# Listed tokens of a fused attention and mixture-of-experts kernel: column groups over strided blocks, 32x32 turns on VectorE

## The chip, the cores and the metric

One core of a Trainium2 chip runs the whole program. The metric is the device time of one execution in microseconds (us); lower is better.

## The reference

Three stages follow each other; the output of each is the input of the next.

```
# 1. attention with a memory term: B=2, H=8, S=576, D=64
a = softmax(causal(q @ k.T / sqrt(D)));  local = a @ v
mem_out = (phi(q) @ M_prev) / (phi(q) . z_prev)
x = g * mem_out + (1 - g) * local            # -> 1152 tokens x 512
# 2. dense layer: w_in 512x2048, w_out 2048x512
h = x @ w_in
g = where(h >= 1, h, where(h <= -1, 0, (h + 1)**2 / 4))
x2 = g @ w_out                               # 1152 x 512
# 3. experts, one per token: w1 8x512x1024, w2 8x1024x512, capacity 288 tokens each
e = argmax(x2 @ w_gate);  gate = max(softmax(x2 @ w_gate))
out[i] = gate * (relu(x2[i] @ w1[e]) @ w2[e])   # tokens over an expert's capacity give 0
```

## The kernel before

Activations are held with features on the 128 partitions and tokens along the free side. Stage 1 goes over 8 pairs of heads, stage 2 over four chunks of 288 tokens, each of eight steps of two 128-feature tiles. The products of the first chunk, and of the expert that runs first, are made of three FP32R products each (high and low parts); the others are plain FP32.

With these inputs nearly all tokens choose one expert, that of token 0. Its first 288 tokens are the first chunk, and they go through that expert as a block: `main_first` (w1) and `main_second` (w2), eight tiles `f` each, in lines 2076 to 2097. The tokens that chose another expert are few. Their numbers come out of a small product (`list_tokens`, line 2127) as a list of up to 32, and these are the "listed tokens". They are computed again from their attention result in rows of 32:

- `all_slots` apart, the queue of GpSimd (POOL) fetches the 32 rows of 512 numbers from `x_d` in device memory (line 844). `x_d` was written earlier by `store_rows` (line 605), by 32x32-turned pieces.
- `few_x` (line 2143) turns the 32x512 rows to four 128x32 tiles with TensorE; ScalarE (ACT) copies them to `x_fewT`.
- `few_hidden` (line 2151) multiplies by `w_in`. The 32 tokens are the stationary operand, 128x32, and the weights stream past. The array is used in four column groups of 32: group `g` writes partitions 32g to 32g+31 of a bank. Group `g` takes the columns 512g to 512g+511 of the 2048, so that all four groups run side by side.
- VectorE (DVE) and ACT apply the piecewise function to the 128x512 result (lines 1634, 1091, 1092, 1636).
- `few_turned` (line 2161) turns it with four TensorE transposes, and ACT copies the result to `g_fewT` (line 1094).
- The product with `w_out` (line 2187) has a quarter of the 2048 contraction rows in each group, 512 columns wide, so that four partial sums lie on the four groups of 32 partitions. DVE copies them (line 1640), and TensorE sums the four and turns them with `sel`, four identities of 32 stacked (line 2196). DVE copies that to `x2_fewT`.
- For three experts `k` (the first one and two others): `few_first` (w1, group g takes the columns 256g to 256g+255 of 1024), ACT's ReLU with the gate (zero for tokens of another expert), `few_turn` (two TensorE transposes), ACT's copy to `h_fewT`, `few_second` (w2, group g takes the columns 128g to 128g+127), all three experts summed in one bank.
- DVE copies the bank to `y_few` and POOL scatters it to the output in pieces of 128 columns (line 875).

The order of all this is written out by hand in each engine's instruction stream. On TensorE `few_x` stands after `main_second(4)`, `few_hidden` after `main_second(5)`, `few_turned` in the middle of `main_second(7)`, and the rest at the end, with the turns of the block's result (`expert_rows`, line 2099) for the first 288 tokens put in between. On the sync engine (SP) the weights of the second other expert are requested once `few_hidden` has ended (line 629).

A part for more than two other experts or more than 32 listed tokens (`work`) is skipped at run time by a count in a register; with these inputs it does not run.

Of the kernel before, what the change touches and what calls it, by code (L numbers as in the profile page):

```python
# [4 lines left out]
F32 = mybir.dt.float32  # L5
F32R = mybir.dt.float32r
BF16 = mybir.dt.bfloat16
I32 = mybir.dt.int32
# [5 lines left out]
def build_program(nc, q, k, v, m_prev, z_prev, beta, w_in, w_out, w_gate, w1, w2, out, capacity):  # L14
# [13 lines left out]
    N = B * S  # L28
# [26 lines left out]
    with ctx:  # L55
# [155 lines left out]
        few_row, _, _ = sb("few_row", [FEW, 1], I32)  # L211
# [33 lines left out]
        x_few, _, _ = sb("x_few", [FEW, DM], F32)  # L245
# [5 lines left out]
        g_fewT, _, _ = sb("g_fewT", [P, FG, P], F32)  # L251
# [3 lines left out]
        x2_few, _, _ = sb("x2_few", [P, DM], F32)  # L255
        x2_fewT, _, _ = sb("x2_fewT", [P, DT, FEW], F32)
        h_few = [sb(f"h_few{k}", [P, F_PART], F32)[0] for k in range(OTHERS + 1)]
        h_fewT = [sb(f"h_fewT{k}", [P, 2, P], F32)[0] for k in range(OTHERS + 1)]
# [130 lines left out]
        s_fpos = sem("s_fpos")  # L389
        s_fx = sem("s_fx")  # L390
        s_ft = sem("s_ft")
# [6 lines left out]
        s_fgt = sem("s_fgt")  # L398
# [5 lines left out]
        s_kt2 = sem("s_kt2")  # L404
# [124 lines left out]
        def _(sp):  # L529
# [75 lines left out]
            def store_rows(j):  # L605

                sp.wait_ge(s_xre, j + 1)
                b, m = divmod(j, KT)
                for a in range(4):
                    sp.dma_start(x_d[b * S:(b + 1) * S, m * P + 32 * a:m * P + 32 * a + 32].rearrange("(g t) c -> t g c", t=32),  # L610
                                 x_rows[j % 2][32 * a:32 * a + 32, :].rearrange("t (g c) -> t g c", c=32)).then_inc(s_xst[j % 2], 16)
# [60 lines left out]
        k_banks = ((bank_pt[0], bank_pt[1], bank_t), (f_bank[0], f_bank[1], f_bank[2]))  # L672
# [11 lines left out]
        def _(pool):  # L684
# [156 lines left out]
            for n in range(2):  # L841
                pool.wait_ge(s_xst[n], 16 * 4 * NPAIR // 2)
            pool.wait_ge(s_fid, 1)
            pool.indirect_dma_start(out=x_few[:, :], out_offset=None, in_=x_d[:, :],
                                    in_offset=bass.IndirectOffsetOnAxis(ap=few_row[:, 0:1], axis=0),
                                    bounds_check=N - 1, oob_is_err=False).then_inc(s_fx, 16)
# [35 lines left out]
        def _(act):  # L882
# [205 lines left out]
            act.wait_ge(s_ft, 1)  # L1088
            act.activation(x_fewT[:, :, :], bank_t[:, 128:256].rearrange("p (m w) -> p m w", w=FEW), ACT.Copy).then_inc(s_fte, 1)
# [3 lines left out]
            act.wait_ge(s_fgt, 1)  # L1093
            act.activation(g_fewT[:, :, :], bank_pt[1][:, :].rearrange("p (b w) -> p b w", w=P), ACT.Copy).then_inc(s_fgte, 1)
# [3 lines left out]
            def few_relu(k):  # L1098

                act.wait_ge(s_kh, k + 1)  # L1100
                act.wait_ge(s_fid, 6)
                act.activation(h_few[k][:, :], k_banks[0][k][:, 0:F_PART], ACT.Relu, scale=few_gate[:, k:k + 1]).then_inc(s_khe, 1)

            def few_turned(k):

                act.wait_ge(s_kt2, k + 1)
                act.activation(h_fewT[k][:, :, :], k_banks[1][k][:, 0:F_PART].rearrange("p (b w) -> p b w", w=P),
                               ACT.Copy).then_inc(s_kte, 1)
# [3 lines left out]
            for k in range(OTHERS + 1):  # L1112
                few_turned(k)
# [15 lines left out]
        def _(dve):  # L1129
# [173 lines left out]
            def clear_counts():  # L1303
# [6 lines left out]
                dve.tensor_copy(parts[:, :, 4:5].rearrange("p r a -> p (r a)"), tok_f[:, 0:1].to_broadcast([ST, NTOK])).then_inc(s_seen, 1)  # L1310
                dve.tensor_reduce(sel[:, :], ident[:, :].rearrange("p (g w) -> p w g", w=32), AX.X, ALU.add
# [283 lines left out]
            def rows_out(J, gates):  # L1595

                for r in range(slot_tiles):
                    dve.wait_ge(s_er, slot_tiles * J + r + 1)
                    dve.tensor_scalar(y_row[r][:, :], row_banks[r][0:ST, :], gates(r), None, ALU.mult).then_inc(s_ere, 1)

            dve.wait_ge(s_list, 1)
# [15 lines left out]
            for g in range(GROUPS):  # L1617
                dve.tensor_scalar(few_t[FEW * g:FEW * (g + 1), :], tab_tok[FEW * g:FEW * (g + 1), :], float(GROUPS), float(g - NOWHERE),
                                  ALU.mult, ALU.add).then_inc(s_fpos, 1)
# [8 lines left out]
            dve.wait_ge(s_fpos, GROUPS)  # L1628
# [45 lines left out]
        def _(pe):  # L1674
# [468 lines left out]
            def few_x():  # L2143

                pe.wait_ge(s_fx, 16)
                for m in range(KT):
                    last = pe.transpose(bank_t[:, 128 + m * FEW:128 + (m + 1) * FEW], x_few[:, m * P:(m + 1) * P],
                                        ident[0:FEW, 0:FEW])
                last.then_inc(s_ft, 1)

            def few_hidden():
# [9 lines left out]
            def few_turned():  # L2161

                pe.wait_ge(s_fg, 1)
                for b in range(FG):
                    last = pe.transpose(bank_pt[1][:, b * P:(b + 1) * P], g_few[:, b * P:(b + 1) * P], ident[:, :])
                last.then_inc(s_fgt, 1)
# [6 lines left out]
            for f in range(ET - 1):  # L2173
# [12 lines left out]
            assert FT == 4 * GROUPS  # L2186
# [102 lines left out]
```

## Time and profile before

| | us |
|---|---|
| median of 3 runs (310.83 to 311.3) | 310.91 |
| the profiled execution | 310.3 |
| its span, first to last instruction in the trace | 308.4 |
| TensorE (PE) busy | 301.0 (98%) |
| PE weight load (PEld) busy | 247.6 (80%) |
| VectorE (DVE) busy | 216.1 (70%) |
| ScalarE (ACT) busy | 153.0 (50%) |
| GpSimd (POOL) busy | 136.5 (44%) |

The profiled execution took 310.3 us, of which 1.9 us lie outside the span. The mean TensorE clock granted was 0.997 of full speed. L2190 in a row is line 2190 of the kernel before. A plain FP32 product appears as two MATMUL records, so that the 16 products of line 2190 are x32.

### The profile page before, as it was taken

Reading aid. Unit: us, or ns where it says so; the run is one execution under the profiler, and the core shown is the slowest. Engines: PE = TensorE matmul, PEld = TensorE weight load, DVE = VectorE, ACT = ScalarE, POOL = GpSimd, SP = SyncE. Lnnn points to the kernel's source line nnn. Section 1 sums busy time; section 2 is a strip of 40 time slices with the busy share of each in tenths; the row PEclk is TensorE's granted clock in tenths of the full one; section 3 lists DMA queues with packets and bytes.
Section 4 is the critical chain, followed back from the end, with each engine's and each line's share of the span. In section 5 each row is a group of like instructions: output and inputs, shape, how many; then the busy total and the mean of one; then the engine's idle time right before and its main releaser. Section 6 shows DMA issues by size and latency. Waiting matters only on the chain.

```text
span 308.4 us, 7108 instructions
## 1 busy us (share of the span) xinstructions
PE 301.0 (98%) x2747; PEld 247.6 (80%) x2747; DVE 216.1 (70%) x574; ACT 153.0 (50%) x337; POOL 136.5 (44%) x154
## 2 busy tenths in 40 slices
PE   7999999999999999999999999999999999999993
PEld 6666676666677988887999989898989899995573
DVE  2999998999977366997884567956775588852300
ACT  1796875867866144655551353446354556301130
POOL 4878997998997300564781012014021333110121
PEclk9999999999999999999999999999999999999998
DMA  7989897861447600000000409660025039079940
GB/s 162 156 192 235 205 207 157 199 187 31 154 119 183 197 2 0 2 2 0 2 0 8 71 3 351 213 98 3 0 38 79 2 99 429 19 255 378 402 145 9
DMA packets 75047, 38.48 MB, mean 125 GB/s; under 512 B 66008, under 2 KB 66016, under 8 KB 73988
## 3 DMA queue, kind: packets, MB, share of 16 engines
q1 hardware_dynamic: 72340, 36.74, 44.9%
q10 hardware_dynamic: 2416, 0.59, 0.9%
q0 software_dynamic: 256, 0.67, 0.7%
q8 instruction: 23, 0.38, 0.5%
q14 instruction: 12, 0.10, 0.1%
HBM read 32.66 MB, written 5.39 MB: 123 GB/s over the span
## 4 chain that ended last, share of the span: by engine, by line
PE 94%; POOL 2%; DVE 1%; issue 1%; ACT 0%; POOLq 0%
PE bank_a L1846 17%; PE bank_b L1846 17%; PE bank_out L1803 6%; PE bank_a L1702 4%; PE bank_b L1906 4%; PE bank_pt L1906 4%; PE bank_pt L1754 4%; PE bank_a L1780 3%; PE bank_out L1800 2%; PE bank_a L2085 2%; PE bank_out L1879 2%; PE bank_b L2085 2%; PE bank_b L1697 2%; PE bank_out L2225 2%; PE bank_b L2095 2%; PE bank_a L2095 2%
## 5 line engine op out<-in xcount | busy, mean ns | idle before, releaser
L722 POOL TENSOR_SCALAR prob<-prob,rl,gate_loc 128x512 f32<-128x512 f32 (+3 forms) x64 | 41.5, 663 | 11.0 <-DVE rl L1243 11.0
L1846 PE MATMUL bank_a<-x_hi,win_hi 128*128 128x288 f32 x128 | 39.3, 307 | 0.0
L1846 PE MATMUL bank_b<-x_hi,win_hi 128*128 128x288 f32 x128 | 38.2, 298 | 0.0
L1846 PE MATMUL bank_b<-x_lo,win_hi 128*128 128x288 f32 x128 | 38.1, 297 | 0.0
L1846 PE MATMUL bank_b<-x_hi,win_lo 128*128 128x288 f32 x128 | 38.0, 297 | 0.0
L1846 PE MATMUL bank_a<-x_hi,win_lo 128*128 128x288 f32 x128 | 38.0, 297 | 0.0
L1846 PE MATMUL bank_a<-x_lo,win_hi 128*128 128x288 f32 x128 | 38.0, 297 | 0.0
L973 ACT ACTIVATE g_raw<-bank_a,biases 128x576 f32<-128x576 f32 x16 | 11.9, 742 | 49.5 <-DVE sq L1320 49.5
L910 ACT ACTIVATE prob<-prob,negmax 128x512 f32<-128x512 f32 (+3 forms) x64 | 35.0, 550 | 0.3 <-DVE negmax L1193 0.3
L806 POOL TENSOR_TENSOR w_lo<-w_sb,w_hi 128x512 fp32r<-128x512 f32 x8 | 11.3, 1414 | 48.3 <-ACT w_hi L1016 48.3
L751 POOL TENSOR_TENSOR x_lo<-xT,x_hi 128x1152 fp32r<-128x1152 f32 x4 | 10.6, 2661 | 48.7 <-ACT x_hi L923 48.7
L1326 DVE TENSOR_TENSOR g_raw<-g_raw,sq 128x576 f32<-128x576 f32 x32 | 31.5, 985 | 0.5 <-ACT sq L974 0.5
L1846 PEld LDWEIGHTS bank_a<-x_hi,win_hi 128*128 128x128 f32 x128 | 24.2, 189 | 3.5 <-issue 3.4
L1320 DVE TENSOR_SCALAR sq<-bank_a 128x576 f32<-128x576 f32 x16 | 12.0, 752 | 21.2 <-PE bank_a L1846 21.2
L819 POOL TENSOR_TENSOR wo_lo<-wout,wo_hi 128x512 fp32r<-128x512 f32 x16 | 22.1, 1392 | 10.5 <-ACT wo_hi L989 10.5
L1846 PEld LDWEIGHTS bank_b<-x_hi,win_hi 128*128 128x128 f32 x128 | 24.2, 189 | 0.5 <-issue 0.5
L974 ACT ACTIVATE sq<-sq,biases 128x576 f32<-128x576 f32 x32 | 24.5, 766 | 0.0
L1846 PEld LDWEIGHTS bank_a<-x_lo,win_hi 128*128 128x128 f32 x128 | 24.1, 189 | 0.0
L1846 PEld LDWEIGHTS bank_b<-x_lo,win_hi 128*128 128x128 f32 x128 | 24.1, 188 | 0.0
L1846 PEld LDWEIGHTS bank_a<-x_hi,win_lo 128*128 128x128 f32 x128 | 24.1, 188 | 0.0
L1846 PEld LDWEIGHTS bank_b<-x_hi,win_lo 128*128 128x128 f32 x128 | 24.1, 188 | 0.0
L973 ACT ACTIVATE g_raw<-bank_b,biases 128x576 f32<-128x576 f32 x16 | 11.9, 741 | 20.1 <-DVE sq L1320 20.1
(333 smaller groups left out, 796.7 us busy)
## 6 DMA issues: line engine op xcount, KB each, us to landing
w_sb<-in_moe_w_dram SPq DMA_DIRECT2D x6, 2048.0 KB, 11.2
win_raw<-in_moe_w_in_dram SPq DMA_DIRECT2D x4, 1024.0 KB, 5.7
wout<-in_moe_w_out_dram SPq DMA_DIRECT2D x4, 1024.0 KB, 5.5
win_raw<-in_moe_w_in_dram SPq DMA_DIRECT2D x1, 4096.0 KB, 13.3
out_dram<-zero_row SPq DMA_DIRECT2D x8, 288.0 KB
x_d<-x_rows SPq DMA_DIRECT2D x32, 72.0 KB, 2.1
v_sb<-in_v_dram SPq DMA_DIRECT2D x16, 128.0 KB, 2.5
qn<-in_q_dram SPq DMA_DIRECT2D x24, 72.0 KB, 5.4
```

The source lines that it names most:

```text
L722: pool.tensor_scalar(prob[u][:, h, :], prob[u][:, h, :], rl[:, c:c + 1], gate_loc[:, 2 * j + h:2 * j + h + 1], ALU.mult, ALU.mult).then_in ...
L819: pool.tensor_tensor(wo_lo[:, f % WSLOTS, :], wout[:, f, :], wo_hi[:, f % WSLOTS, :], ALU.subtract).then_inc(s_wol, 1)
L910: last = act.activation(p, p, ACT.Exp, scale=-1.0, bias=negmax[:, c:c + 1], accum_out=rsum[:, c:c + 1])
L973: act.activation(g_raw[:, 2 * d:2 * d + 2, :], h_bank(d), ACT.Relu, bias=biases[:, 1:2]).then_inc(s_re, 1)
L974: act.activation(sq[d % 2][:, :, :], sq[d % 2][:, :, :], ACT.Square, scale=0.5, bias=biases[:, 0:1]).then_inc(s_sq, 1)
L1326: dve.tensor_tensor(g_raw[:, two, :], g_raw[:, two, :], sq[d % 2][:, :, :], ALU.add).then_inc(s_g, 1)
L1702: last = pe.matmul(s_part(u, h), qT[i % 2][part, u * P:(u + 1) * P], kT[i % 2][part, 0:(u + 1) * P], start=True, stop=True)
L1754: last = pe.transpose(dst[:, c * P:(c + 1) * P], prob[u][:, h, c * P:(c + 1) * P], ident[:, :])
L1803: last = pe.matmul(bank_t[part, c * P:NFULL * P], v_sb[j % 2][:, c, h, :], probT[:, h, c * KSTEP + c * P:c * KSTEP + NFULL * P], start=Fal ...
L1846: last = pe.matmul(h_bank(d)[:, t, :], w[:, m, f:f + P], x[c % 2][:, m, :], start=(m == 0 and n == 0), stop=(m == KT - 1 and n == 2))
L1906: last = pe.matmul(y_bank[m], w[:, f % WSLOTS, part], x, start=(f == 0 and n == 0), stop=(f == FT - 1 and n == 2))
L2085: last = pe.matmul(e_bank(f)[:, 0:SLOTS], w, x[:, m, :], start=(m == 0 and n == 0), stop=(m == DT - 1 and n == 2))
```

## The change

What it does, for the listed tokens alone:

- A column group `g` no longer takes a contiguous quarter of the columns, but every fourth run of 32 columns: the runs g, g+4, g+8 and so on. `strided()` gives this view of the moving operand, and the bank is written contiguously as before. If a 128-partition result of this form is turned in 32x32 blocks, it stands directly with the contraction features on the partitions.
- So the three TensorE turns (`few_x`, `few_turned`, `few_turn`) and the sum with `sel` go. In their place come 32x32-block transposes by VectorE: `x_fewT` (128x128), `g_fewT` (128x512), `x2_fewT` (128x128, from PSUM) and three of `h_fewT` (128x256). The ACT copies go too.
- The product with `w_out` has all 16 tiles of the contraction in every group and 128 columns in each, in place of 4 tiles and 512 columns: 64 products of 128 columns in place of 16 of 512.
- The fetch of the rows reads 128 pieces of 128 numbers in place of 32 rows of 512, with index 4 * token + group (`of_group`, made by eight small memsets while the first chunk runs). `few_t` is one instruction in place of four. For the block order to come out, `store_rows` writes its 32-column pieces to other columns of `x_d`.
- On TensorE the three tiles of `expert_rows` stand together behind the product with `w_out`.
- `work` turns its rows by four times as many products (not run here).

```diff
@@ SP, store_rows
-                    sp.dma_start(x_d[b * S:(b + 1) * S, m * P + 32 * a:m * P + 32 * a + 32].rearrange("(g t) c -> t g c", t=32),
+                    sp.dma_start(x_d[b * S:(b + 1) * S, a * P + 32 * m:a * P + 32 * m + 32].rearrange("(g t) c -> t g c", t=32),
@@ POOL
-            pool.indirect_dma_start(out=x_few[:, :], out_offset=None, in_=x_d[:, :],
+            quarters = x_d.rearrange("n (a w) -> (n a) w", a=GROUPS)
+            pool.indirect_dma_start(out=x_few[:, :], out_offset=None, in_=quarters[:, :],
                                     in_offset=bass.IndirectOffsetOnAxis(ap=few_row[:, 0:1], axis=0),
-                                    bounds_check=N - 1, oob_is_err=False).then_inc(s_fx, 16)
+                                    bounds_check=GROUPS * N - 1, oob_is_err=False).then_inc(s_fx, 16)
@@ ACT
-            act.wait_ge(s_ft, 1)
-            act.activation(x_fewT[:, :, :], bank_t[:, 128:256].rearrange("p (m w) -> p m w", w=FEW), ACT.Copy).then_inc(s_fte, 1)
...
-            act.wait_ge(s_fgt, 1)
-            act.activation(g_fewT[:, :, :], bank_pt[1][:, :].rearrange("p (b w) -> p b w", w=P), ACT.Copy).then_inc(s_fgte, 1)
...
-            for k in range(OTHERS + 1):
-                few_turned(k)
@@ DVE, first chunk
+                for g in range(GROUPS):
+                    for n, value in enumerate((float(g), float(g - NOWHERE))):
+                        dve.memset(of_group[FEW * g:FEW * (g + 1), n:n + 1], value).then_inc(s_group, 1)
@@ DVE, listed tokens
-            dve.scalar_tensor_tensor(out=few_row[:, :], in0=tab_few[0:FEW, 3:4], scalar=float(ST), in1=tab_few[0:FEW, 4:5],
-                                     op0=ALU.mult, op1=ALU.add).then_inc(s_fid, 1)
             dve.scalar_tensor_tensor(out=tab_tok[:, :], in0=tab_few[:, 3:4], scalar=float(ST), in1=tab_few[:, 4:5],
                                      op0=ALU.mult, op1=ALU.add).then_inc(s_tab, 1)
+            dve.wait_ge(s_tab, 2)
+            dve.scalar_tensor_tensor(out=few_row[:, :], in0=tab_tok[:, :], scalar=float(GROUPS), in1=of_group[:, 0:1],
+                                     op0=ALU.mult, op1=ALU.add).then_inc(s_fid, 1)
...
+            dve.wait_ge(s_fx, 16)
+            dve.transpose(x_fewT[:, :, :].rearrange("p m w -> p (m w)"), x_few[:, :]).then_inc(s_fte, 1)
             dve.wait_ge(s_fh, 1)
             dve.tensor_scalar(c_few[:, :], bank_pt[0][:, :], -1.0, 1.0, ALU.max, ALU.min).then_inc(s_fc, 1)
             dve.wait_ge(s_fsq, 1)
             dve.tensor_tensor(g_few[:, :], g_few[:, :], c_few[:, :], ALU.add).then_inc(s_fg, 1)
+            dve.wait_ge(s_fg, 1)
+            dve.transpose(g_fewT[:, :, :].rearrange("p t w -> p (t w)"), g_few[:, :]).then_inc(s_fgte, 1)
             copy_yt(0, 0)
             copy_yt(0, 1)
             dve.wait_ge(s_f2, 1)
-            dve.tensor_copy(x2_few[:, :], bank_o[:, :]).then_inc(s_f2e, 1)
+            dve.transpose(x2_fewT[:, :, :].rearrange("p m w -> p (m w)"), bank_o[:, 0:P]).then_inc(s_f2e, 1)
-            row_out(0)
-            dve.wait_ge(s_f2, 2)
-            dve.tensor_copy(x2_fewT[:, :, :], f_bank[3][:, 0:P].rearrange("p (m w) -> p m w", w=FEW)).then_inc(s_f2e, 1)
-            for r in range(1, slot_tiles):
+            for r in range(slot_tiles):
                 row_out(r)
+            for k in range(OTHERS + 1):
+                dve.wait_ge(s_khe, k + 1)
+                dve.transpose(h_fewT[k][:, :, :].rearrange("p f w -> p (f w)"), h_few[k][:, :]).then_inc(s_kte, 1)
@@ PE
+            def strided(w, g):
+                return w.rearrange("p (t g c) -> p g t c", g=GROUPS, c=FEW)[:, g, :, :]
 
             def few_hidden():
...
-                        last = pe.matmul(bank_pt[0][FEW * g:FEW * (g + 1), :], x_fewT[:, m, :], win_raw[:, m, DM * g:DM * (g + 1)],
-                                         start=(m == 0), stop=(m == KT - 1))
+                        last = pe.matmul(bank_pt[0][FEW * g:FEW * (g + 1), :].rearrange("p (t c) -> p t c", c=FEW), x_fewT[:, m, :],
+                                         strided(win_raw[:, m, :], g), start=(m == 0), stop=(m == KT - 1))
...
-                if f == 4:
-                    few_x()
...
-            main_second(ET - 1, range(2))
-            few_turned()
-            main_second(ET - 1, range(2, DT))
+            main_second(ET - 1, range(DT))
             pe.wait_ge(s_fgte, 1)
-            for i in range(FT // GROUPS):
+            for f in range(FT):
                 for g in range(GROUPS):
-                    f = GROUPS * i + g
-                    last = pe.matmul(bank_o[FEW * g:FEW * (g + 1), :], g_fewT[:, f % FG, FEW * (f // FG):FEW * (f // FG + 1)],
-                                     wout[:, f, :], start=(i == 0), stop=(i == FT // GROUPS - 1))
+                    last = pe.matmul(bank_o[FEW * g:FEW * (g + 1), 0:P].rearrange("p (t c) -> p t c", c=FEW), g_fewT[:, f, :],
+                                     strided(wout[:, f, :], g), start=(f == 0), stop=(f == FT - 1))
             last.then_inc(s_f2, 1)
-            expert_rows(0, range(2))
+            expert_rows(0, range(slot_tiles))
             pe.wait_ge(s_f2e, 1)
-            for m in range(DT):
-                last = pe.matmul(f_bank[3][:, FEW * m:FEW * (m + 1)], x2_few[:, m * P:(m + 1) * P], sel[:, :], start=True, stop=True)
-            last.then_inc(s_f2, 1)
-            pe.wait_ge(s_fid, 2)
-            expert_rows(0, range(2, slot_tiles))
-            pe.wait_ge(s_f2e, 2)
...
-                        last = pe.matmul(k_banks[0][k][FEW * g:FEW * (g + 1), 0:F_PART], x2_fewT[:, m, :],
-                                         w1_sb[k][:, m, F_PART * g:F_PART * (g + 1)], start=(m == 0), stop=(m == DT - 1))
+                        last = pe.matmul(k_banks[k][FEW * g:FEW * (g + 1), 0:F_PART].rearrange("p (t c) -> p t c", c=FEW),
+                                         x2_fewT[:, m, :], strided(w1_sb[k][:, m, :], g), start=(m == 0), stop=(m == DT - 1))
...
-            for k in range(OTHERS + 1):
-                few_turn(k)
```

## Rows read from the trace of the kernel before

**Rows 1.** The page's chain that ended last, share of the span by engine.

```profile
PE 94%; POOL 2%; DVE 1%; issue 1%; ACT 0%; POOLq 0%
```

**Rows 2.** The chain in order of time from 262 us on: start us, us, what.

```profile
275.81 0.36 PE bank_out L2147 x4
276.17 0.99 PE bank_a L2095 x6
277.17 0.80 PE bank_b L2095 x6
277.97 3.62 PE bank_pt L2157 x32
...
281.61 0.70 DVE c_few L1634
...
282.33 0.69 ACT g_few L1091
...
283.66 0.70 DVE g_few L1636
...
284.41 0.66 PE bank_pt L2165 x4
285.07 0.80 PE bank_b L2095 x6
285.86 3.57 PE bank_out L2190 x32
289.43 1.01 PE bank_a L2104 x8
290.44 0.89 PE bank_b L2196 x8
291.33 0.45 PE bank_b L2104 x4
291.78 3.59 PE bank_pt L2207 x64
295.37 1.73 PE bank_out L2207 x32
297.10 0.59 PE bank_a L2216 x4
...
297.69 0.44 PE bank_b L2216 x2
298.13 5.59 PE bank_out L2225 x192
...
303.75 0.30 DVE y_few L1653
```

**Rows 3.** TensorE's timeline: start us, us, engine line, tiles.

```profile
285.79 3.64 PE L2190 MATMUL bank_out<-wout,g_fewT 128*32 128x512 f32 x32
```

**Rows 4.** VectorE's groups by form: busy us, mean ns, idle before.

```profile
L1337 DVE STREAM_TRANSPOSE w_turn<-wout 128x1024 f32<-128x1024 f32 x8 | 9.8, 1229 | 0.0
...
L1348 DVE STREAM_TRANSPOSE wp<-bank_out 128x512 f32<-128x512 f32 x1 | 0.7, 703 | 0.0
```

**Rows 5.** SP's timeline from 255 us on: start of the last weight requests.

```profile
281.74 0.37 SPq L599 DMA_DIRECT2D w_sb<-in_moe_w_dram  x1
282.21 0.46 SPq L603 DMA_DIRECT2D w_sb<-in_moe_w_dram  x1
```

**Rows 6.** Tile w_sb from 255 us on: the four requests' time to landing.

```profile
DMA to landing us min/median/max: 8.6/11.4/14.2
```

**Rows 7.** DMA issues, 220 to 309 us: median us to landing.

```profile
x_few<-x_d,few_row POOLq DMA_INDIRECT x1, 3.3
```

**Rows 8.** POOL's timeline: the fetch of the listed rows.

```profile
269.01 1.60 POOL L844 DMA_INDIRECT x_few<-x_d,few_row  x1 [11.70 <-DVE few_row L1604]
```

**Rows 9.** VectorE's timeline in the first chunk.

```profile
112.14 0.06 DVE L1306 MEMSET seen<- 96x4 uint32 x1
...
115.49 0.76 DVE L1320 TENSOR_SCALAR sq<-bank_a 128x576 f32<-128x576 f32 x1 [0.49 <-PE bank_a L1846]
```

More of the change, by code:

```diff
@@ L210, in build_program @@
         few_id, _, _ = sb("few_id", [P, 1], I32)
-        few_row, _, _ = sb("few_row", [FEW, 1], I32)
+        few_row, _, _ = sb("few_row", [P, 1], I32)
+        of_group, _, _ = sb("of_group", [P, 2], F32)
         job_id, _, _ = sb("job_id", [ST, NR], I32)
@@ L244, in build_program @@
         hT, _, _ = sb("hT", [P, ET, SLOTS], F32, at=phase)
-        x_few, _, _ = sb("x_few", [FEW, DM], F32)
+        x_few, _, _ = sb("x_few", [P, DM_PART], F32)
         x_fewT, _, _ = sb("x_fewT", [P, KT, FEW], F32)
@@ L250, in build_program @@
         c_few, _, _ = sb("c_few", [P, DM], F32)
-        g_fewT, _, _ = sb("g_fewT", [P, FG, P], F32)
+        g_fewT, _, _ = sb("g_fewT", [P, FT, FEW], F32)
         assert offset[0] <= reused
@@ L254, in build_program @@
         y_row = [sb(f"y_row{r}", [ST, DM], F32)[0] for r in range(slot_tiles)]
-        x2_few, _, _ = sb("x2_few", [P, DM], F32)
         x2_fewT, _, _ = sb("x2_fewT", [P, DT, FEW], F32)
         h_few = [sb(f"h_few{k}", [P, F_PART], F32)[0] for k in range(OTHERS + 1)]
-        h_fewT = [sb(f"h_fewT{k}", [P, 2, P], F32)[0] for k in range(OTHERS + 1)]
+        h_fewT = [sb(f"h_fewT{k}", [P, ET, FEW], F32)[0] for k in range(OTHERS + 1)]
         assert offset[0] <= later_at
@@ L389, in build_program @@
         s_fpos = sem("s_fpos")
+        s_group = sem("s_group")
         s_fx = sem("s_fx")
-        s_ft = sem("s_ft")
         s_fte = sem("s_fte")
@@ L397, in build_program @@
         s_fg = sem("s_fg")
-        s_fgt = sem("s_fgt")
         s_fgte = sem("s_fgte")
@@ L403, in build_program @@
         s_khe = sem("s_khe")
-        s_kt2 = sem("s_kt2")
         s_kte = sem("s_kte")
@@ L670, in s_part @@
             return s_bank(u)[:, 512 * h + at:512 * h + at + (u + 1) * P]
-        k_banks = ((bank_pt[0], bank_pt[1], bank_t), (f_bank[0], f_bank[1], f_bank[2]))
+        k_banks = (bank_pt[0], bank_pt[1], bank_t)
         NGROUP = DM // P
@@ L1101, in few_relu @@
                 act.wait_ge(s_fid, 6)
[L1102 to L1108, printed above, removed]
+                act.activation(h_few[k][:, :], k_banks[k][:, 0:F_PART], ACT.Relu, scale=few_gate[:, k:k + 1]).then_inc(s_khe, 1)
             for k in range(OTHERS + 1):
                 few_relu(k)
-            for k in range(OTHERS + 1):
-                few_turned(k)
             def work(n):
@@ L1599, in rows_out @@
                     dve.tensor_scalar(y_row[r][:, :], row_banks[r][0:ST, :], gates(r), None, ALU.mult).then_inc(s_ere, 1)
+            dve.wait_ge(s_group, 2 * GROUPS)
             dve.wait_ge(s_list, 1)
@@ L1616, in _ @@
             dve.wait_ge(s_tab, 3)
-            for g in range(GROUPS):
-                dve.tensor_scalar(few_t[FEW * g:FEW * (g + 1), :], tab_tok[FEW * g:FEW * (g + 1), :], float(GROUPS), float(g - NOWHERE),
-                                  ALU.mult, ALU.add).then_inc(s_fpos, 1)
+            dve.scalar_tensor_tensor(out=few_t[:, :], in0=tab_tok[:, :], scalar=float(GROUPS), in1=of_group[:, 1:2],
+                                     op0=ALU.mult, op1=ALU.add).then_inc(s_fpos, 1)
             second_lo(6)
@@ L1627, in _ @@
             dve.wait_ge(s_fid, 4)
-            dve.wait_ge(s_fpos, GROUPS)
+            dve.wait_ge(s_fpos, 1)
             dve.tensor_tensor(few_at[:, :], few_any[:, :], few_t[:, :], ALU.mult).then_inc(s_fid, 1)
@@ L2141, in name_jobs @@
                 pe.matmul(sum_ps, biases[0:E, 1:2], col[:, 4:6], start=True, stop=True).then_inc(s_name, 1)
[L2143 to L2149, printed above, removed]
+            def strided(w, g):
+                return w.rearrange("p (t g c) -> p g t c", g=GROUPS, c=FEW)[:, g, :, :]
             def few_hidden():
@@ L2156, in few_hidden @@
                     for g in range(GROUPS):
-                        last = pe.matmul(bank_pt[0][FEW * g:FEW * (g + 1), :], x_fewT[:, m, :], win_raw[:, m, DM * g:DM * (g + 1)],
-                                         start=(m == 0), stop=(m == KT - 1))
+                        last = pe.matmul(bank_pt[0][FEW * g:FEW * (g + 1), :].rearrange("p (t c) -> p t c", c=FEW), x_fewT[:, m, :],
+                                         strided(win_raw[:, m, :], g), start=(m == 0), stop=(m == KT - 1))
                 last.then_inc(s_fh, 1)
[L2161 to L2166, printed above, removed]
             pe.wait_ge(s_xh, 1)
@@ L2206, in few_first @@
                     for g in range(GROUPS):
-                        last = pe.matmul(k_banks[0][k][FEW * g:FEW * (g + 1), 0:F_PART], x2_fewT[:, m, :],
-                                         w1_sb[k][:, m, F_PART * g:F_PART * (g + 1)], start=(m == 0), stop=(m == DT - 1))
+                        last = pe.matmul(k_banks[k][FEW * g:FEW * (g + 1), 0:F_PART].rearrange("p (t c) -> p t c", c=FEW),
+                                         x2_fewT[:, m, :], strided(w1_sb[k][:, m, :], g), start=(m == 0), stop=(m == DT - 1))
                 last.then_inc(s_kh, 1)
-            def few_turn(k):
-                pe.wait_ge(s_khe, k + 1)
-                pe.wait_ge(s_ere, k + 1)
-                for b in range(2):
-                    last = pe.transpose(k_banks[1][k][:, b * P:(b + 1) * P], h_few[k][:, b * P:(b + 1) * P], ident[:, :])
-                last.then_inc(s_kt2, 1)
             def few_second(k):
@@ L2225, in few_second @@
                         last = pe.matmul(bank_o[FEW * g:FEW * (g + 1), 0:DM_PART],
-                                         h_fewT[k][:, f % 2, FEW * (f // 2):FEW * (f // 2 + 1)],
+                                         h_fewT[k][:, f, :],
                                          w2_sb[k][:, f, DM_PART * g:DM_PART * (g + 1)],
@@ L2244, in work @@
                     for m in range(KT):
-                        last = pe.transpose((bank_pt[0], bank_pt[1], bank_t)[r][:, m * ST:(m + 1) * ST],
-                                            job_rows[:, r, m * P:(m + 1) * P], ident[0:ST, 0:ST])
+                        for a in range(GROUPS):
+                            last = pe.matmul((bank_pt[0], bank_pt[1], bank_t)[r][32 * a:32 * a + 32, m * ST:(m + 1) * ST],
+                                             job_rows[:, r, a * P + 32 * m:a * P + 32 * m + 32], ident[0:ST, 0:ST],
+                                             start=True, stop=True)
                     last.then_inc(s_jt, 1)
```

1 line of the change is left out of this document (removed).

## The prediction, written before the changed kernel ran

> **What bounds the kernel now.** I read the page's chain of waits first: 94% of the span hangs on TensorE [rows 1], so a TensorE instruction that goes saves its time unless something else is late in its place. Then the same chain in order of time from 262 us on [rows 2]. There the listed tokens are threaded through the block's products (line 2095), and from 285.86 us they are nearly alone. The reader is to see four things: the three places where TensorE turns (lines 2147, 2165, 2216), the sum with `sel` (line 2196), the one stretch where the chain leaves TensorE (DVE, ACT, ACT, DVE from 281.61 to 284.4), and that each product block starts where the one before it ends, so that no weights are waited for. Last, the landing of the late weight requests [rows 5, 6], because a TensorE that comes sooner may meet them.
>
> All moments below are those of the profiled execution: it took 310.3 us, 308.4 of them span. The median of the runs is 310.91. I work out a difference on the former and take it off the latter.
>
> **Part 1: `few_x` goes.** Line 2147 has 0.36 us, and the block product behind it takes 0.99 where its neighbour of the same six records takes 0.80 [rows 2]. Removed: 0.36 + 0.19 = 0.55 us. `x_fewT` now comes from a DVE transpose of 128x128. `few_hidden` wants it at 277.97 - 0.55 = 277.4. The fetch starts at 269.01 and lands 3.3 later, at 272.3 [rows 7, 8]. An additional DVE instruction ahead of it (of 0.3 at most, which is what DVE needs for 128x128 at the end of rows 2) and the transpose bring that to 273. It is hidden by 4 us of block products. The fetch has 128 pieces in place of 32. Between no dearer (272.3) and four times 3.3, 13.2 (282.2, 4.8 late), I take the former, as the bytes are the same; the latter is a rival below.
>
> **Part 2: `few_hidden` and the function.** It keeps 16 products of 512 columns in four groups, 3.62 us [rows 2], if reading runs of 32 columns costs nothing (rival S). It then ends 0.55 earlier, and `c_few` starts at 281.06. The chain DVE, ACT, ACT, DVE is unchanged: `g_few` starts 283.66 - 281.61 = 2.05 later, at 283.11. New behind it is a DVE transpose of 128x512. From one operation to its dependent takes 282.33 - 281.61 = 0.72, so it starts at 283.83. Its cost: 703 ns from PSUM for that size, 1229 for twice the size from SBUF [rows 4]. Half of 1229 is 0.61, all of it 1.23; I take 0.70. With 0.04 to hand over, `g_fewT` is there at 284.57.
>
> TensorE has meanwhile done all of `main_second(7)` in one go. The last product of `few_hidden` ends at 277.97 + 3.62 - 0.55 = 281.04; the first six records at 0.99 and three times 0.80 make 3.39, so it is free at 284.43. So `few_turned` (0.66 and its place in the middle of the block) costs nothing any more, and TensorE waits some 0.15 us for the transpose. This is the one new wait; queued behind it are all remaining products, and behind the transpose on DVE two copies of the block's result, which are wanted 3.8 us later.
>
> **Part 3: the product with `w_out`.** Before: 8 rounds of four groups with 512 columns in 3.57 us, 0.446 each. After: 32 rounds with 128 columns. Line 2225 is of that form: 192 records, 48 rounds in 5.59, 0.116 each [rows 2]. 32 x 0.116 = 3.73, so 0.16 more. The bounds are 0 (the same columns stream in all) and 0.5 (each of the 96 additional records at 5 ns). The row of before reads 3.64 from 285.79 [rows 3], so it ends at 289.43; after it ends at 284.57 + 3.64 + 0.16 = 288.37. Gained to here: 1.06.
>
> **Part 4: the sum goes.** Line 2196, 0.89 us [rows 2], goes. The three tiles of rows stay: 1.01 + 0.45 = 1.46. Under them DVE turns the bank's 128x128, about 0.3 as the copy of that size at 303.75 [rows 2], in place of a 128x512 copy and a second one. It is done near 288.8 and wanted at 288.37 + 1.46 = 289.83. Hidden, with 1 us of cover; without the cover it would cost 0.4. `few_first` starts at 289.83, before at 291.78. Gained to here: 1.95.
>
> **Part 5: `few_first`, then no turn.** 96 records in 3.59 + 1.73 = 5.32 [rows 2], unchanged, to 295.15. Then 297.10 to 298.13, the two `few_turn` pieces, go: 1.03 more. `few_second(0)` wants its transpose at 295.15, made from a product that ended at 289.83 + 1.8 = 291.6; ReLU and transpose of 128x256 cost less than 0.7 each, which is what 128x512 costs DVE and ACT [rows 2]. DVE first has three row tiles, under 0.8 each by the nearest large operations of rows 2, until about 291.2. Hidden. The last, k = 2, is made by 295.15 + 1.4 = 296.6 and wanted two thirds into `few_second`, at 295.15 + 32 x 0.116 = 298.9. Hidden by 2.3 us.
>
> The products on both sides now have the same form, and block 2225 loses the slow entry that a change of form brings (0.99 against 0.80 [rows 2]). Bounds 0 and 0.25; I take 0.10.
>
> **Part 6: the rest.** Eight memsets of about 0.06 us in the first chunk [rows 9] are 0.5 us on DVE. The next clip had waited 0.49 for TensorE there, so they fit to within 0.02. `few_t` loses three instructions, in cover as well. The stores to `x_d` write the same number of 128-byte pieces to other places: I take 0, between 0.1 either way, as they run under block products. The skipped `work` costs nothing.
>
> **Weights.** SP asks for the third expert's weights when `few_hidden` ends, at 281.74 and 282.21 [rows 5]. The slowest request of all took 14.2 [rows 6], so w2 is there at 296.4 at the latest. The w1 request goes first and is among the quicker two, below the median of 11.4: 293.1 at the latest, 290.3 at the earliest. `few_first(2)` now starts at 289.83 + 3.59 = 293.4, `few_second(2)` at 298.9. Both are still in time, the first by 0.3 to 3.1 us, the second by 2.5.
>
> **The sum.** 1.06 (to the end of the `w_out` product) + 0.89 + 1.03 + 0.10 = 3.08 us. Span 308.4 to 305.3, profiled execution 310.3 to 307.2, median 310.91 - 3.08 = **307.8 us**.
>
> **Rivals.**
>
> S, the strided stream is slow (the slower side). From `few_hidden` to `few_first` every product reads its moving operand in runs of 32 numbers that lie 128 numbers apart. On TensorE no row shows such a read. It would bear on 3.62 + 3.73 + 5.32 = 12.7 us of products, all on the path. It eats the gain from 3.08 / 12.7 = 24% slower on, and at half rate the time is 307.8 + 12.7 = 320.5. Against it speaks that DVE reads `wout` in runs of 32 at 1229 / 1024 = 1.20 ns per number, no slower than a contiguous 703 / 512 = 1.37 [rows 4]. For it: nothing in the profile, but TensorE reads four streams at once.
>
> The Trainium skill has the rule for it. "Advanced Engine Details and Errata", section "Memory Cachelines", has SBUF in lines of 16 bytes, with full speed if following accesses stay in a line, and says of PSUM, in lines of 8 bytes, that "Any non-contiguous AP significantly slows down matmuls". Taken for any operand, that sentence is rival S. Taken by the lines it is no loss, since a run of 128 bytes fills whole lines and the bank is written contiguously. No row of before decides it.
>
> W, something new is waited for and eats about half. Either w1 of the third expert comes after 293.4 (its bound is 0.3 us away, and the scatters of the block's rows now start 1.9 us sooner, into the same transfers), or the 128x512 transpose takes the 1.23 of the twice larger one (0.5 late). With 0.5 for the transpose and 0.8 for the weights the gain is 3.08 - 1.3 = 1.8: 309.1 us. For it: the transfers run without a gap in that time. Against: the bounds are the worst that rows 6 allow.
>
> F, the fetch costs four times as much per piece: `few_hidden` starts 4.8 late, 307.8 + 4.8 = 312.6. Against it: the bytes are the same, and 3.3 us is long for 64 KB, so it is latency and not pieces.
>
> **How the numbers follow.** Forecast 0.78 (own range 307.2 to 308.5, from the bounds 0.09 better and 0.5 worse on the transpose, 0.16 better and 0.35 worse on part 3, 0.15 better and 0.10 worse on part 5, and 0.3 of run to run), W 0.12 at 309.1, S 0.08 with 320.5 at its middle, F 0.02 at 312.6. A difference of less than 0.2% (0.62 us) I call none. Faster takes the forecast and nearly all of W, 0.88; none takes the rest of W and an S of about 20 to 28%, 0.04; slower takes most of S and F, 0.08. The range that leaves out 2 in 10 reaches down to 306.9 and up over most of W to 309.3.
>
> **What would show it.** Part 1: no line-2147 records and six-record pieces of 0.80 there. Part 2: the chain goes c_few, g_few, g_few again, g_fewT, then the `w_out` product, with a TensorE wait of 0.1 to 0.4. Part 3: 128 records in about 3.8. Parts 4 and 5: three row tiles of 1.5, then 96 and 192 records with no gap. S would show as rounds in `few_hidden` above 0.45 us. The prediction is wrong if the new time is above 309.3: then S, if those rounds are longer, or a wait ahead of the third `few_first` or of `few_hidden`.

## The result and the profile after

The changed kernel took 307.9 us (median of 6 runs, 306.46 to 308.89) against 310.86 for the kernel before on the same chip (median of 6): ratio 0.9912, 95% interval 0.9895 to 0.9929. The profiled execution took 307.44 us, 305.3 of them span. The forecast was 307.8.

The chain of the changed kernel in order of time from 262 us on (start us, us, what), to be read beside [rows 2]:

```profile
277.04 3.62 PE bank_pt L2148 x32
...
280.68 0.70 DVE c_few L1627
...
282.74 0.70 DVE g_few L1629
...
283.46 0.72 DVE g_fewT L1631
...
284.23 3.70 PE bank_out L2168 x128
287.93 1.01 PE bank_a L2099 x8
288.94 0.44 PE bank_b L2099 x4
289.38 3.59 PE bank_pt L2179 x64
292.97 1.73 PE bank_out L2179 x32
294.69 2.17 PE bank_out L2189 x76
296.86 0.41 issue
297.28 3.49 PE bank_out L2189 x116
...
300.79 0.30 DVE y_few L1648
```

Lines 2147, 2165, 2196 and 2216 of before are gone. `few_hidden` and `few_first` keep their length, 3.62 and 3.59 + 1.73, and the `w_out` product takes 3.70 (3.57 before). One thing has no counterpart in [rows 2]: a hole of 0.41 us, "issue", after record 76 of the last block, where TensorE waits for nothing that the profile shows. Because of it and slow records beside it, the last block, `few_second`, takes 6.08 us (294.69 to 300.77) where it took 5.59.

TensorE's timeline, the new wait ahead of the `w_out` product:

```profile
284.23 3.70 PE L2168 MATMUL bank_out<-wout,g_fewT 128*32 128x128 f32 x128 [0.23 <-DVE g_fewT L1631]
```

SP's last request and its landing, w2 of the third expert (us, last column):

```profile
281.28 0.46 SPq L601 DMA_DIRECT2D w_sb<-in_moe_w_dram  x1
...
w_sb<-in_moe_w_dram SPq DMA_DIRECT2D x1, 2048.0 KB, 16.6
```

It came at 281.28 + 16.6 = 297.9. The slowest of before took 14.2 [rows 6]. The w1 request ahead of it took 10.8 us from 280.81, so w1 came at 291.6, and the third part of `few_first` wants it at 289.38 + 3.59 = 293.0. The scatters of the rows took 5.6 us to land (median of three; 3.7 before).

### The profile page after: what moved, and what is told of

Read it like the earlier page. It is cut to its first block, busy times and chain, and to the rows that moved or that the text cites. A ratio compares the mean times of both kernels' runs of the same rounds, so it can differ in the third digit from the quotient of the medians.

```text
span 305.3 us, 7256 instructions
## 1 busy us (share of the span) xinstructions
PE 297.8 (98%) x2821; PEld 247.5 (81%) x2821; DVE 217.4 (71%) x583; ACT 151.4 (50%) x332; POOL 136.4 (45%) x154
## 4 chain that ended last, share of the span: by engine, by line
PE 94%; POOL 2%; DVE 1%; issue 1%; ACT 0%; POOLq 0%
PE bank_a L1841 17%; PE bank_b L1841 17%; PE bank_out L1798 6%; PE bank_a L1697 4%; PE bank_b L1901 4%; PE bank_pt L1901 4%; PE bank_pt L1749 4%; PE bank_a L1775 3%; PE bank_out L1795 2%; PE bank_a L2080 2%; PE bank_out L1874 2%; PE bank_b L2080 2%; PE bank_b L1692 2%; PE bank_out L2189 2%; PE bank_out L1786 2%; PE bank_a L2090 2%
```

## The experiments

Each kernel is the changed one with the edit shown (`...` stands for lines left out), except e8_before_short and e11_before_again, which are the kernel before; ratios are to the kernel before, run on the same chip at the same time. "The two blocks" are `few_first` and `few_second` without what stands between them; the best seen is 5.32 + 5.28 = 10.60 us. What a trace takes above that is called the stall below; a hole is a piece of it in which TensorE stands idle.

**e0_again**: the changed kernel, no edit.

> The changed kernel once more, for its scatter and for the hole of 0.41 us in the last product block (after record 76 of 192). If the hole belongs to this program (where its instructions or transfers lie), it is in this trace too, at the same record and of 0.3 to 0.6 us. If it is chance, it is at another record or absent, and the block then takes 5.6 us in place of 6.07. Time 307.9, within 0.5.

Measured: 307.77 us, ratio 0.9891 (0.987 to 0.9911). Its chain:

```profile
289.55 3.88 PE bank_pt L2179 x63
...
293.65 0.84 PE bank_out L2179 x10
294.49 0.09 issue
294.58 1.19 PE bank_out L2179 x17
...
295.98 5.34 PE bank_out L2189 x186
```

The stall is there, but it begins in the other block: the first 63 records of `few_first` take 3.88 us, where 64 took 3.59, and the records behind them are slower still. The two blocks end at 301.32, 11.77 us after their start, 1.17 above the best. So it is neither tied to record 76 nor absent. The same program has it in two places.

**e1_contiguous**: no strided read. Each group streams a contiguous quarter, so other columns are multiplied and the listed tokens' result is another; number and size of the products are kept.

```diff
-                return w.rearrange("p (t g c) -> p g t c", g=GROUPS, c=FEW)[:, g, :, :]
+                return w.rearrange("p (g t c) -> p g t c", g=GROUPS, c=FEW)[:, g, :, :]
```

> The changed kernel, but each column group streams a contiguous quarter of the columns, so that wrong columns are multiplied; number and size of all products are kept. Theory F (a moving operand in runs of 32 numbers costs nothing): few_hidden stays at 3.62 us, the w_out product at 3.70, few_first at 5.32, the time at 307.9 within 0.4. Rival S (the strided read costs something): these three blocks, 12.6 us together, get shorter by the part that it costs; at 2% that is 0.25 us, at 10% 1.3 us, time 306.6.

Measured: 308.03 us, ratio 0.9895 (0.9878 to 0.9912). The three blocks that had read in runs of 32:

```profile
276.96 3.62 PE bank_pt L2148 x32
...
284.15 3.70 PE bank_out L2168 x128
...
289.30 3.59 PE bank_pt L2179 x64
292.89 0.63 PE bank_out L2179 x9
293.52 0.09 issue
```

The first two blocks and the first two thirds of the third are the same to a hundredth. The last third of `few_first` holds the stall in this trace, 11.75 us for the two blocks, so the stall needs no strided read. With the strided read and no stall there, the changed kernel's trace has 5.32 for the whole block, as the contiguous one of before had. Nor is the time shorter than that of e0_again on the same chip (307.77). Rival S is out: the strided read is free in all three widths (512, 128 and 256 columns).

**e2_turn_h**: `h` turned by TensorE and copied by ACT as before. `few_first` reads contiguous quarters again and `few_second` takes its slices from the other layout (both not shown below).

```diff
+            for k in range(OTHERS + 1):
+                few_turned(k)
...
-            for k in range(OTHERS + 1):
-                dve.wait_ge(s_khe, k + 1)
-                dve.transpose(h_fewT[k][:, :, :].rearrange("p f w -> p (f w)"), h_few[k][:, :]).then_inc(s_kte, 1)
...
+            for k in range(OTHERS + 1):
+                few_turn(k)
```

> One part undone: h is turned by TensorE and copied by ACT as before (few_first reads contiguous quarters again), all else as changed. Theory F: the two pieces of turns come back, 1.03 us, and nothing else, so the last block starts 1.0 us later. If the hole of 0.41 us in the last block comes from transfers that are still under way, a block that starts 1.0 us later has no hole or a smaller one: time 307.9 + 1.0 - 0.4 = 308.5. If the hole is tied to the instruction count, it moves by the twelve records more and stays at 0.4: 308.9. Rival (the turns were hidden and gave nothing): 307.9.

Measured: 309.32 us, ratio 0.9932 (0.9918 to 0.9946). The turns are back:

```profile
294.59 0.29 issue
294.88 1.50 PE bank_out L2185 x21
296.38 0.59 PE bank_a L2194 x4
296.97 0.42 PE bank_b L2194 x2
297.39 5.42 PE bank_out L2203 x192
```

0.59 + 0.42 = 1.01 us, as the term of the prediction had it. Against e0_again of the same chip the time is 1.55 us longer, and 0.4 above even the 308.9 of the expectation. The two traces, 1.48 us apart at `y_few`, show where it is: 1.01 for the turns, 0.17 more of stall, and 0.31 by which this trace is behind where `main_second` begins. The rival that the turns were hidden and gave nothing (307.9) is out. The stall is in `few_first` here (6.52 for 5.32), so a start of the last block 1 us later did not remove it; the expectation that it shrinks fell.

**e4_no_w2**: w2 of the third expert is not requested; its product reads the second expert's w2 in its place.

```diff
-            second_weights(2, others[1])
...
-                pe.wait_ge(s_wf[k], 16)
+                pe.wait_ge(s_wf[min(k, 1)], 16)
```

> The changed kernel without the request for the third expert's w2 (its product reads the second expert's), 2 MB less of traffic at the end. Theory D (the hole of 0.41 us in the last block comes from transfers under way at 294 to 298 us): the hole goes, the block takes 5.6 us in place of 6.07, time 307.4. Theory I (the hole is in how the instruction stream is laid out, whatever the traffic): hole and 307.9 stay. Theory W (the w2 landing at 297.9 is what holds it): the hole goes as in D, and it goes at the third expert's records too.

Measured: 308.7 us, ratio 0.99 (0.9884 to 0.9917). The stall stays, 11.81 us for the two blocks, most of it in `few_first` in this trace. The landing of w2 is not its cause.

**e3_sum**: the `w_out` product and the sum as before, with DVE's two copies (not shown below).

```diff
-            for f in range(FT):
-                for g in range(GROUPS):
-                    last = pe.matmul(bank_o[FEW * g:FEW * (g + 1), 0:P]..., g_fewT[:, f, :], strided(wout[:, f, :], g), ...)
+            for i in range(FT // GROUPS):
+                for g in range(GROUPS):
+                    last = pe.matmul(bank_o[FEW * g:FEW * (g + 1), :], g_fewT[:, GROUPS * i + g, :], wout[:, GROUPS * i + g, :], ...)
...
+            for m in range(DT):
+                last = pe.matmul(f_bank[3][:, FEW * m:FEW * (m + 1)], x2_few[:, m * P:(m + 1) * P], sel[:, :], start=True, stop=True)
```

> One part undone: the w_out product is again 16 products of 512 columns (32 records in place of 128), with DVE's 128x512 copy, the sum with sel on TensorE and the copy to x2_fewT; all else as changed. Theory F, from the terms of the prediction: the sum comes back with 0.89 us and the product gets 0.13 shorter, so the last-but-one block (few_first) starts 0.76 us later. On top of that the stall that all traces of the changed form show in few_first or few_second (0.7 to 1.3 us in the two blocks together, above 5.32 + 5.34 us), and the kernel before does not (0.25). Theory I (the stall follows from a long run of short records, TensorE's instruction stream arriving too slowly): 96 records fewer ahead of it, so the two blocks take 10.9 us as before and the time is 307.8 + 0.76 - 0.8 = 307.8. Theory P (the stall belongs to the time at which the rows are scattered): it stays, and the time is 308.6.

Measured: 307.55 us, ratio 0.9919 (0.9903 to 0.9936).

```profile
284.22 3.64 PE bank_out L2172 x32
287.86 1.01 PE bank_a L2103 x8
288.87 0.88 PE bank_b L2178 x8
289.75 0.46 PE bank_b L2103 x4
290.21 3.59 PE bank_pt L2188 x64
293.80 1.73 PE bank_out L2188 x32
295.53 5.28 PE bank_out L2198 x192
```

From the start of the `w_out` product to `few_first` it takes 5.99 us, the changed one 5.15 (284.23 to 289.38). So the term of parts 3 and 4 is 0.84 us. And there is no stall at all: 10.60 for the two blocks. Its `few_first` starts 0.83 later than in the changed kernel's trace and its last block ends only 0.04 later (300.81 for 300.77).

**e7_scatter_late**: the rows are scattered after the last block.

```diff
+            pool.wait_ge(s_kye, 1)
             for r in range(slot_tiles):
                 pool.wait_ge(s_ere, r + 1)
```

> The changed kernel, but POOL scatters the three row tiles only after the last product block (this adds some 4 us at the end, so only the blocks are compared). Theory P (scatters of the rows, with their traffic at 293 to 296 us, stall TensorE): few_first and few_second take 5.32 and 5.34, 10.7 together. Theory I (instruction stream): the two blocks still take 11.4 to 11.8.

Measured: 311.49 us, ratio 1.0051 (1.0032 to 1.007), of which only the blocks count. The hole is after record 76 again:

```profile
294.79 2.17 PE bank_out L2190 x76
296.96 0.28 issue
297.24 3.49 PE bank_out L2190 x116
```

11.26 us for the two blocks. The scatters are not the cause. What the time shows beside: held back, they move the last scatter from 301.90 to 305.67 us.

**e5_hidden_4** and **e6_hidden_3**: `few_hidden` sooner, by one block product (shown) and by two (`f == 3`).

```diff
-                if f == 5:
+                if f == 4:
                     few_hidden()
```

> The changed kernel with few_hidden one block product earlier, behind main_second(4). The chain DVE, ACT, ACT, DVE, DVE behind it then has two block products of cover, so TensorE's wait of 0.23 us ahead of the w_out product goes, and the third expert's weights are asked for 1.6 us sooner. Time 307.8 - 0.2 = 307.6. If the weights' landing mattered (landing at 297.6 against a want at 298.2), the stall in the two last blocks would shrink too: 306.8.

> As before it, but few_hidden two block products earlier, behind main_second(3), at 273.9 us, where x_fewT was ready at 273.6. As the one before: 307.6; if DVE makes x_fewT later than TensorE is there, up to 0.3 us of wait comes in ahead of few_hidden: 307.9.

Measured: 307.18 us, ratio 0.9908 (0.9889 to 0.9927), and 307.31, ratio 0.9909 (0.9891 to 0.9927). The chain of e5_hidden_4 never leaves TensorE any more:

```profile
275.48 3.57 PE bank_pt L2148 x32
...
284.06 3.63 PE bank_out L2168 x128
```

From the start of `few_hidden` to the `w_out` product: 8.58 us with two more pieces of 0.80 in it, against 7.19 in the changed kernel; 0.21 less for the same work. That is the wait of 0.23, as expected. As a time it is too small for these intervals. In e6_hidden_3 `few_hidden` starts at 274.40 with no wait ahead of it, so `x_fewT` was ready there too. The third expert's w2 was asked for 1.6 and 2.6 us sooner. The two blocks took 11.06 us in the one trace, the least of this form, and 11.39 in the other, as much as in the changed kernel; one trace each doesn't tell this from chance.

**e8_before_short**: the kernel before, its `w_out` product in 64 products of 128 columns.

```diff
+            for n in range(4):
                 for i in range(FT // GROUPS):
...
-                    last = pe.matmul(bank_o[FEW * g:FEW * (g + 1), :], ..., wout[:, f, :], ...)
+                    last = pe.matmul(bank_o[FEW * g:FEW * (g + 1), n * P:(n + 1) * P], ..., wout[:, f, n * P:(n + 1) * P], ...)
```

> The kernel before with one thing of the change alone: its w_out product is cut into 64 products of 128 columns (128 records in place of 32), same sums, same results, no strided read. Theory I (a long run of short records makes TensorE's instruction stream fall behind, and the stall comes 100 to 200 records later): the product itself takes 3.7 in place of 3.57, and few_first to few_second, 11.97 us from start to end before, get 0.5 to 1.1 longer: time of before + 0.6 to 1.2. Theory N (nothing but the records' own time): time of before + 0.13 to 0.16.

Measured: 310.87 us, ratio 1.0002 (0.9988 to 1.0017).

```profile
286.15 3.63 PE bank_out L2191 x128
...
292.13 4.08 PE bank_pt L2210 x64
296.21 0.07 issue
296.28 1.99 PE bank_out L2210 x32
...
299.27 5.42 PE bank_out L2228 x192
```

The trace shows the stall in the kernel before too, once its product has 128 records: `few_first` takes 6.14 for 5.32. The product itself costs 0.06 more, not 0.16. But the timed runs do not show the 0.6 us or more that were expected: the upper end of the interval is 0.53 us. In the trace the theory holds, in the time it does not.

**e9_no_third**: neither weight of the third expert is requested; its products read the second expert's (not shown below).

```diff
-            sp.wait_ge(s_fh, 1)
-            first_weights(2, others[1])
-            second_weights(2, others[1])
```

> The changed kernel without both requests for the third expert's weights (its products read the second expert's), so that no weights move from 285 us on. Theory I with a busy DMA (instructions are fetched through the engines that carry the weights and come late for that): the stall in few_first and few_second goes, 10.7 us for the two blocks, time 306.9 to 307.1. Theory I without it (the fetch is late whatever moves): they take 11.4 to 11.8 and the time is 307.8.

Measured: 307.76 us, ratio 0.9907 (0.9887 to 0.9926).

```profile
289.16 3.59 PE bank_pt L2176 x64
292.75 0.63 PE bank_out L2176 x9
293.38 0.10 issue
```

11.81 us for the two blocks: the stall is there with no weights moving since 285 us. A busy DMA is not needed for it.

**e10_spread**: another order on TensorE. DVE turns `x2_fewT` ahead of its two copies of the block's result to suit it (not shown below).

```diff
-                if f == 5:
+                if f == 3:
                     few_hidden()
-            main_second(ET - 1, range(DT))
             pe.wait_ge(s_fgte, 1)
...
             last.then_inc(s_f2, 1)
-            expert_rows(0, range(slot_tiles))
+            main_second(ET - 1, range(DT))
...
-            for k in range(OTHERS + 1):
+            few_first(0)
+            expert_rows(0, range(slot_tiles))
+            for k in range(1, OTHERS + 1):
```

> The changed kernel in another order on TensorE: few_hidden behind main_second(3), the w_out product ahead of main_second(7) in place of behind it, the row tiles between few_first(0) and few_first(1). All products are kept; the short records now have 24 long ones (3.2 us) behind them. Theory I: with the long ones behind it the stall goes (10.7 us for few_first and few_second without the rows), and TensorE's wait of 0.23 us for g_fewT goes; two more changes of form cost 0.2 to 0.4. Time 307.8 - 0.9 - 0.2 + 0.3 = 307.0. Theory N (the stall belongs to the end of the kernel, whatever stands ahead): 307.8.

Measured: 308.53 us, ratio 0.9925 (0.9905 to 0.9945).

```profile
295.24 0.44 PE bank_out L2188 x8
295.69 1.00 issue
296.69 5.28 PE bank_out L2188 x184
```

A hole of 1.00 us in one piece, after record 8 of the last block. Long records behind the short ones did not help: the two blocks take 12.17 us without the rows, the most of all traces, so theory I fell in the form in which it was put. Theory N, that the stall belongs to the end of the kernel, is not refuted by the place: the hole begins at 295.69 us, between those of the other traces. Its 307.8 us is missed by 0.7, and e3_sum, with the same end and no stall, speaks against it.

**e11_before_again**: the kernel before, no edit.

> The kernel before once more, for a second trace of it. Its first trace has few_first at 5.32 us and few_second at 5.59, 0.25 to 0.3 above the best seen since (5.32 and 5.34). Theory I (the stall comes with the 96 additional records of the changed w_out product): again no hole, 10.9 us for the two blocks at most. Theory C (the stall is there in some executions of any of these kernels): a hole of 0.3 to 1.2 us can be in this trace too; then nothing of the 0.73 to 1.1 us may be charged to the change. Ratio to the kernel before 1.000 either way.

Measured: 310.06 us, ratio 0.9996 (0.9982 to 1.0009).

```profile
291.74 3.59 PE bank_pt L2207 x64
295.33 1.73 PE bank_out L2207 x32
...
298.09 5.42 PE bank_out L2225 x192
```

No hole, 10.74 for the two blocks. Over all traces: with 128 records in the `w_out` product eleven of eleven have a stall (0.46 to 1.57 us above 10.60), with 32 records there is no hole in any of three, and they are 0, 0.14 and 0.31 above it. From 0.31 to 0.46 is a small step, so the split rests on the holes as much as on the sums.

## Why the prediction was right, point by point

- **Part 1, 0.55 us: right.** `few_x` and its slow entry are gone. `x_few` landed 3.3 us after its request as before, so the 128 pieces cost nothing, and rival F is out.
- **Part 2: right.** The chain is c_few, g_few, g_few, g_fewT. The transpose takes 0.72 (taken: 0.70) and TensorE waits 0.23 (said: 0.1 to 0.4). The edit with `few_hidden` sooner shows that this wait is worth 0.21.
- **Part 3: mis-sized by 0.1.** 3.70 against the 3.80 of the prediction. Line 2225, from which the 0.116 a round came, had some slowness of its own in that trace; its form takes 5.28 to 5.42 in others.
- **Part 4, 0.89, and part 5, 1.03: right**, shown by e3_sum (0.84 with the product's own growth of 0.06 in it) and e2_turn_h (1.01). `few_first` starts 2.40 us sooner than in [rows 2]; 1.95 was said. 0.38 of it is not counted as a gain of the change: the trace was that much ahead where `main_second` begins. That start lies between 266.71 and 267.89 us in the eleven traces of the changed form and between 267.25 and 267.58 in the three of the form before, so 0.38 is within its scatter. The first piece there, before and after:

```profile
267.30 0.91 PE bank_a L2095 x6
```

```profile
266.92 0.91 PE bank_a L2090 x6
```

- **Part 5, the last block: wrong.** I took 0.10 off it for its entry. It got 0.49 longer. The entry itself was about right: where no stall is, the block takes 5.28 behind its own form (e3_sum) and 5.42 behind the turns (e11_before_again), 0.14 more. What the prediction did not have is the stall. So in the two traces the listed tokens' part gained 2.6 us (2.96 at `y_few`, less the 0.38) where 3.08 was forecast. The medians are 2.96 apart all the same, so the time came out as forecast with some luck.
- **Part 6: right.** The eight memsets took 0.50 us, and the clip that had waited 0.49 for TensorE [rows 9] started without a wait.
- **Weights: the bound was wrong.** "At 296.4 at the latest" took the slowest landing of before, 14.2, for a limit. It was 16.6, at 297.9, with the third part of the last block wanting it at 297.28 + 52 x 0.03 = 298.8. Cover of 0.9 us, not 2.5. Nothing waited, in this trace. The working had the landing as the request plus a duration, and the traces show it otherwise: in ten of them this w2 was requested at moments from 278.64 to 282.21 us and landed between 296.4 and 297.9, after 14.2 to 18.6 us. A sooner request did not bring it sooner. The scatters did not make it late either: held back in e7_scatter_late, it took 16.0. For w1 the bounds held (291.6 and 1.4 us of cover, said: 0.3 to 3.1).
- **The range.** The parts named for it add up to 0.70 better and 1.25 worse, 307.1 to 309.1; the upper end of 308.5 was taken narrower than that without a word. The measured 307.9 lies in both.
- **Rivals.** S is refuted by e1_contiguous. The Trainium skill's page "Advanced Engine Details and Errata", section "Memory Cachelines", has its sentence on non-contiguous patterns under PSUM, and it can't be taken for every operand: reading SBUF in runs of 128 bytes did not slow a product (3.62 and 3.70 us with and without in e1_contiguous, 5.32 after and before). All these products write PSUM contiguously, so no run tests the sentence where it stands. W did not occur as described: w1 was in time and the transpose took 0.72. Something of a little over half its size did in the changed kernel's trace (0.79 us of stall against the 1.3 of W), by another mechanism. F is out, as said under part 1.

**What stays open.** In the traces the stall comes with the greater number of records (e3_sum takes it away, e8_before_short brings it into the kernel before), and it does not come from the strided read, the scatters, w2, or weight traffic. It is not the clock: the granted clock is 1.00 in every microsecond from 266 to 302 us of all fourteen traces. No run separates the number of the records from where they put the rest of the instruction stream. That TensorE's instructions arrive late is my guess for it. It would fit that the weight loads stood idle as well in the changed kernel's trace, for 0.68 us ahead of the load at 297.27, with nothing that the profile shows to wait for. But no run shows it, and e10_spread speaks against the simple form of it. The transfers of the instruction queue don't settle it: they start near 288.6, 294.8 and 298.2 us in the changed kernel and near 292.6, 296.6 and 300.2 in e3_sum, and none lies in the hole. Nor do the timed runs show its price: e8_before_short is slower by 0.53 us at the most, and e3_sum, with 0.84 us more of products and no stall, is 0.2 to 0.9 us slower by the ratios than the two measurements of the changed kernel. Whether an execution outside these traces has it in this size was not settled.

None of the versions is faster than the changed kernel by more than the intervals hold. The lowest median is that of e5_hidden_4, 307.18 us, on a chip on which the kernel before took 310.06; its ratio of 0.9908 is that of the changed kernel (0.9912) within the intervals.

## What to carry to other kernels

If an engine bounds the end of a kernel, layouts that leave a result in 32x32-turned form let VectorE do under cover what TensorE would do on the path: here turns and a sum of 2.5 us on the path, for one wait of 0.23. Choose the column order of a product so that the block transpose puts the contraction where the next product wants it; reading the moving operand in runs of 32 numbers was free here. Take a landing time seen once as a sample, not as a bound. Where transfers follow each other without a gap, look at the moment at which they end and not at the time since the request. Count the records that a cut into smaller products adds, not only their columns.

## What the hardware showed that was not expected

- Holes of 0.07 to 1.00 us on TensorE with no releaser, beside rounds that run slow, at changing records, in all eleven traces with 128 records in the `w_out` product and in none of three with 32.
- The same request of 2 MB took 14.2 to 18.6 us in ten traces, the two made soonest taking longest (17.2 and 18.6): it landed between 296.4 and 297.9 us in all of them. The row scatters are not the reason, since it took 16.0 us with them held back.
- Cutting 16 products of 512 columns in four groups into 64 of 128 costs 0.06 us (3.57 to 3.63, e8_before_short), against the 0.16 of the forecast.
